# Rows of x turned on VectorE and carried through memory beside h, in two mixture-of-experts stages after chunked attention

## What is computed

```python
# N, D, E, F = 3072, 512, 8, 1024
top2 = argpartition(-noisy_logits, 2)[:, :2]          # first mixture
for e in range(E):
    for k in range(2):
        mask = top2[:, k] == e
        h = np.maximum(x[mask] @ w1[e], 0.0)
        out[mask] += top2_w[mask, k, None] * (h @ w2[e])
expert_idx = np.argmax(x @ w_gate, axis=1)            # second mixture, x = out of the first
for e in range(E):
    h = np.maximum(x[mask] @ w1[e], 0.0)
    out[mask] = gate_w[mask, None] * (h @ w2[e])
```

## Time and profile before

| | us |
|---|---|
| median of 3 runs | 1158.09 |
| lowest and highest run | 1156.57, 1162.1 |
| profiled execution, its own time | 1158.69 |
| its span in the trace | 1156.6 |

### The profile page before, as it was taken

The page is one execution under the profiler, slowest core; times in us unless marked ns, Lnnn a source line. Parts: engine busy times, 40 slices in busy tenths (PEclk is TensorE's granted clock), DMA queues, the critical chain, the costliest instruction groups (busy, mean ns, idle before and its releaser), DMA issues.

```text
span 1156.6 us, 29685 instructions
## 1 busy us (share of the span) xinstructions
PE 1085.6 (94%) x7939; PEld 879.6 (76%) x7940; DVE 643.4 (56%) x1360; ACT 280.0 (24%) x534; POOL 317.1 (27%) x473
## 2 busy tenths in 40 slices
PE   5989788999999999999999999989889999999995
PEld 4767566788888888888888888856668888878783
DVE  2767585655553552644635536317885246576861
ACT  3566321121212212121212122115211212121111
POOL 2004313332222232333322223220133223333321
PEclk9797889999999999999999999999999999999998
DMA  8998974877685774766867757559387447777952
GB/s 344 357 336 282 329 247 131 242 219 220 184 234 138 216 209 137 221 198 162 244 168 204 222 131 215 137 114 252 100 280 230 141 157 236 236 244 234 306 178 68
DMA packets 126990, 245.87 MB, mean 213 GB/s; under 512 B 17454, under 2 KB 70878, under 8 KB 126960
## 3 DMA queue, kind: packets, MB, share of 16 engines
q1 hardware_dynamic: 48608, 112.38, 28.9%
q10 hardware_dynamic: 61728, 90.25, 24.1%
q0 software_dynamic: 16624, 42.88, 16.7%
HBM read 169.51 MB, written 76.73 MB: 213 GB/s over the span
## 4 chain that ended last, share of the span: by engine, by line
PE 63%; DVE 7%; DMA 6%; issue 5%; DVEq 4%; ACT 1%; ACTq 1%; POOL 1%; POOLq 0%
PE moe_ps_y L1597 10%; PE moe_ps_y L1598 10%; PE moe_ps_y L1602 10%; PE moe_ps_h L1597 10%; PE moe_ps_h L1598 9%; PE moe_ps_h L1602 9%; DMA moe_h_moved<-h_d 3%; PE moe_ps_x L1590 3%; DVE weights L141 2%; DVEq L1478 2%; DMA moe_xg<-x_d,moe_from_row 2%; ACTq L1660 1%; DVE moe_h_lo L1710 1%; DVEq L141 1%; PE g_bank L343 1%
## 5 line engine op out<-in xcount | busy, mean ns | idle before, releaser
L1597 PE MATMUL moe_ps_h<-weights,moe_x_hi 128*128 (+1 forms) x640 | 253.1, 395 | 11.8 <-ACT moe_x_hi L1665 4.9
L1597 PE MATMUL moe_ps_y<-weights,moe_h_hi 128*128 (+1 forms) x624 | 251.5, 403 | 7.0 <-ACT moe_y L1685 3.4
L1598 PE MATMUL moe_ps_h<-weights,moe_x_hi 128*128 (+1 forms) x640 | 251.0, 392 | 0.0
L1598 PE MATMUL moe_ps_y<-weights,moe_h_hi 128*128 (+1 forms) x624 | 244.6, 392 | 0.0
L1710 DVE SCALAR_TENSOR_TENSOR moe_h_lo<-moe_h_moved,moe_h_hi 128x256 fp32r<-128x256 f32 x312 | 111.8, 422 | 231.2 <-ACT moe_h_hi L1674 231.2
L1674 ACT ACTIVATE moe_h_hi<-moe_h_moved 128x1024 fp32r<-128x1024 f32 x78 | 82.8, 1062 | 383.5 <-PE moe_ps_y L1602 313.9
L1602 PE MATMUL moe_ps_h<-weights,moe_x_lo 128*128 (+1 forms) x640 | 171.7, 390 | 0.0
L147 DVE TENSOR_TENSOR weights<-stage,weights (+1 forms) x128 | 156.8, 1225 | 19.7 <-DVE weights L141 19.2
L1602 PE MATMUL moe_ps_y<-weights,moe_h_lo 128*128 (+1 forms) x624 | 154.1, 389 | 0.0
L1597 PEld LDWEIGHTS moe_ps_h<-weights,moe_x_hi 128*128 128x128 f32 x640 | 121.2, 189 | 41.8 <-issue 15.3
L1597 PEld LDWEIGHTS moe_ps_y<-weights,moe_h_hi 128*128 128x128 f32 x624 | 117.8, 189 | 32.4 <-issue 7.1
(11 more groups left out here) (259 smaller groups left out, 861.8 us busy)
## 6 DMA issues: line engine op xcount, KB each, us to landing
stage<-in_w SPq DMA_DIRECT2D x128, 512.0 KB
h_d<-moe_h_turned ACTq DMA_DIRECT2D x80, 512.0 KB
moe_h_moved<-h_d ACTq DMA_DIRECT2D x320, 128.0 KB
v_sb<-in_v SPq DMA_DIRECT2D x24, 520.0 KB, 5.3
k_sb<-in_k SPq DMA_DIRECT2D x24, 512.0 KB, 6.3
x_d<-zero SPq DMA_DIRECT2D x27, 260.0 KB, 7.2
q_sb<-in_q SPq DMA_DIRECT2D x24, 256.0 KB, 4.5
x_d<-x_sb ACTq DMA_DIRECT2D x24, 256.0 KB, 6.0
```

The source lines that it names most:

```text
L1597: pe.matmul(out, a_hi, b_hi, start=(i == 0), stop=False)
L1598: pe.matmul(out, a_hi, b_lo, start=False, stop=False)
```

## The change

The transposes of x on TensorE are dropped from the loop. VectorE turns the rows of tile t+3 in 32x32 blocks from `xg` (`turn_x`) into the last four columns of a wider buffer `turned`, where the two turns of `h` of tile t+1 fill the first eight. The buffer in memory is laid out so that one DMA reads a whole tile back (`fetch`, 128 rows of 6 KB, before 4 x 128 pieces of 1 KB). It is written in four DMAs (`park`), two behind the first turn of h and two behind the second, each of 128 pieces of 1.5 KB. `high_x(t+2)` and `low_x(t+2)` read what `fetch(t)` brought, and `high_x` comes behind `park(t+1)` in ScalarE's order. The gathers run a tile or two further ahead. The first tiles of each mixture keep the transposes of before.

```diff
+TC = FC + DC
+LAG = 5
...
-        self.h_blocks = h_d.rearrange("(a p) (b r) -> b p a r", a=QB, b=QB)
+        self.parts = [h_d[b * QR:(b + 1) * QR, :].rearrange("p (a r) -> a p r", a=QB) for b in range(QB)]
...
-            self.h_turned = sb("h_turned", [P, QB, FC, QR])
-            self.h_moved = sb("h_moved", [P, QB, FC, QR])
+            self.turned = sb("turned", [P, QB, TC, QR])
+            self.moved = sb("moved", [P, QB, TC, QR])
...
-    def park(self, act, t):
+    def park(self, act, t, with_x=False):
...
-        act.wait_ge(s("turned"), t * 2 + 4)
         if not (isinstance(t, int) and t == 0):
-            act.wait_ge(s("moved"), t * (16 * QB))
-        act.dma_start(self.h_d, self.h_turned[:, :, :, :].rearrange("p b c q -> p (b c q)")).then_inc(s("parked"), 16)
...
+            act.wait_ge(s("moved"), t * 16)
+        if with_x:
+            act.wait_ge(s("xt_done"), t + 3)
+        n = TC if with_x else FC
+        for f in range(2):
+            act.wait_ge(s("turned"), t * 2 + (f + 3))
+            for b in (2 * f, 2 * f + 1):
+                act.dma_start(self.parts[b][:, :, 0:n * QR],
+                              self.turned[:, b, 0:n, :].rearrange("p c q -> p (c q)")).then_inc(s("parked"), 16)
...
-        act.wait_ge(s("parked"), t * 16 + 16)
+        act.wait_ge(s("parked"), t * (16 * QB) + 16 * QB)
         if not (isinstance(t, int) and t == 0):
             act.wait_ge(s("h_split"), t)
-        for b in range(QB):
-            act.dma_start(self.h_moved[b * QR:(b + 1) * QR, :, :, :].rearrange("p a c q -> p a (c q)"),
-                          self.h_blocks[b]).then_inc(s("moved"), 16)
...
+        if with_x:
+            act.wait_ge(s("x_split"), t + 2)
+        n = TC if with_x else FC
+        act.dma_start(self.moved[:, :, 0:n, :].rearrange("p a c q -> p a (c q)"),
+                      self.h_d.rearrange("p (a r) -> p a r", a=QB)[:, :, 0:n * QR]).then_inc(s("moved"), 16)
...
+        if moved:
+            act.wait_ge(s("moved"), t * 16 - 16)
+            act.wait_ge(s("l1_done"), t * 2)
+            act.nop(nofuse=True)
+            act.activation(self.x_hi[:, :, :].rearrange("p c (a q) -> p c a q", a=QB),
+                           self.moved[:, :, FC:TC, :].rearrange("p a c q -> p c a q"), ACT.Copy)\
+               .then_inc(s("x_high"), 1)
...
+    def turn_x(self, dve, t, second=False):
+
+        s, xg = self.s, self.xg_b if second else self.xg
+        if second:
+            dve.wait_ge(s("gathered_b"), 32)
+        else:
+            dve.wait_ge(s("gathered"), t * 16 - 16)
+        dve.wait_ge(s("parked"), t * (16 * QB) - 2 * 16 * QB)
+        dve.nop(nofuse=True)
+        dve.transpose(self.turned[:, :, FC:TC, :].rearrange("p b c q -> p c b q"),
+                      xg[:, 0:DM].rearrange("p (c b q) -> p c b q", c=DC, b=QB)).then_inc(s("xt_done"), 1)
...
             self.splits(dve, frm, mid)
+            if not first and not end:
+                self.turn_x(dve, t + 3)
             self.turn(dve, t + 1)
-            self.low_x(dve, t + 2)
+            if not end:
+                self.low_x(dve, t + 2, moved=not first)
+            if first:
+                self.turn_x(dve, t + 3, second=True)
             self.splits(dve, mid, to)
             self.low_h(dve, t, end)
...
-            self.high_x(act, t + 2)
-            self.park(act, t + 1)
+            if first:
+                self.high_x(act, t + 2)
+            self.park(act, t + 1, with_x=not end)
+            if not first and not end:
+                self.high_x(act, t + 2, moved=True)
             self.high_h(act, t, end=end)
             self.weigh(act, t - 1)
-            self.fetch(act, t + 1)
...
+            self.fetch(act, t + 1, with_x=not end)
...
             self.first_product(pe, t + 1)
-            self.x_transposes(pe, t + 2)
             self.second_product(pe, t - 1)
...
-    def pool_loop(self, pool, begin, m):
+    def pool_loop(self, pool, m):
...
+            self.scatter(pool, t)
+            pool.wait_ge(s("xt_done"), t + (LAG + 1))
             pool.nop(nofuse=True)
-            self.keep_gate(pool, t + 3)
-            self.gather(pool, t + 4)
-            self.scatter(pool, t)
...
+            self.keep_gate(pool, t + LAG)
+            self.gather(pool, t + (LAG + 1))
```

More of the change, by code:

```diff
@@ L611, in _ @@
             x.gather(pool, 0)
-            for t in range(1, EARLY):
-                pool.wait_ge(s("xt_done"), t)
-                x.keep_gate(pool, t - 1)
-                x.gather(pool, t)
+            x.gather(pool, 1, second=True)
+            pool.wait_ge(s("xt_done"), 1)
+            x.keep_gate(pool, 0)
+            x.gather(pool, 2)
+            pool.wait_ge(s("xt_done"), 2)
+            x.keep_gate(pool, 1, second=True)
             store_gates(2)
@@ L625, in _ @@
             x.scatter(pool, 0)
-            m = x.tiles(pool)
-            pool.wait_ge(s("xt_done"), EARLY + 1)
-            x.keep_gate(pool, EARLY)
-            x.gather(pool, EARLY + 1)
-            x.pool_loop(pool, 1, m)
+            m = x.gathered_ahead(pool)
+            pool.wait_ge(s("xt_done"), 4)
+            x.keep_gate(pool, 3)
+            x.gather(pool, 4)
+            x.gather(pool, 5, second=True)
+            pool.wait_ge(s("xt_done"), 5)
+            x.keep_gate(pool, 4)
+            x.gather(pool, 6)
+            pool.wait_ge(s("gathered_b"), 32)
+            x.keep_gate(pool, 5, second=True)
+            x.pool_loop(pool, m)
             pool.sem_inc(sem("x2_whole"), 1)
@@ L805, in _ @@
             ranks(2, NT)
-            x.x_transposes(pe, 1)
+            x.x_transposes(pe, 1, second=True)
             x.first_product(pe, 1)
@@ L1587, in x_transposes @@
         else:
-            pe.wait_ge(self.s("gathered"), t * 16 + (16 if isinstance(t, int) and t == 0 else self.gathers))
+            pe.wait_ge(self.s("gathered"), max(t, 1) * 16)
         for cc in range(DC):
@@ new lines, in high_x @@
+    def high_x(self, act, t, moved=False):
+        s = self.s
+        if moved:
[6 more added lines that the diff above has]
+        else:
+            act.wait_ge(s("xt_done"), t + 1)
+            act.activation(self.x_hi[:, :, :], self.ps_x[:, :, :], ACT.Copy).then_inc(s("x_high"), 1)
@@ L1686, in weigh, with low_x @@
            .then_inc(s("y_ready"), 1)
-    def low_x(self, dve, t):
+    def low_x(self, dve, t, moved=False):
         dve.wait_ge(self.s("x_high"), t + 1)
-        dve.tensor_tensor(self.x_lo[:, :, :], self.ps_x[:, :, :], self.x_hi[:, :, :].bitcast(F32), ALU.subtract)\
-           .then_inc(self.s("x_split"), 1)
+        if moved:
+            last = dve.tensor_tensor(self.x_lo[:, :, :].rearrange("p c (a q) -> p c a q", a=QB),
+                                     self.moved[:, :, FC:TC, :].rearrange("p a c q -> p c a q"),
+                                     self.x_hi[:, :, :].bitcast(F32).rearrange("p c (a q) -> p c a q", a=QB),
+                                     ALU.subtract)
+        else:
+            last = dve.tensor_tensor(self.x_lo[:, :, :], self.ps_x[:, :, :], self.x_hi[:, :, :].bitcast(F32),
+                                     ALU.subtract)
+        last.then_inc(self.s("x_split"), 1)
     def turn(self, dve, t):
@@ L1709, in low_h @@
             cols = slice(a * QR, (a + 1) * QR)
-            last = dve.scalar_tensor_tensor(out=h_lo[:, :, cols], in0=self.h_moved[:, a, :, :], scalar=0.0,
+            last = dve.scalar_tensor_tensor(out=h_lo[:, :, cols], in0=self.moved[:, a, 0:FC, :], scalar=0.0,
                                             in1=h_hi[:, :, cols].bitcast(F32), op0=ALU.max, op1=ALU.subtract)
@@ L1728, in vector_loop, with tile @@
         s, before, middle = self.s, self.routes.before, self.routes.middle
-        def tile(t, end=False):
+        def tile(t, first=False, end=False):
             frm, mid, to = self.counts(dve, t, (before, t), (middle, t), (before, t + 1))
@@ L1756, in scalar_loop, with tile @@
     def scalar_loop(self, act, begin, m):
-        def tile(t, end=False):
-            self.high_x(act, t + 2)
-            self.park(act, t + 1)
+        def tile(t, first=False, end=False):
+            if first:
[3 more added lines that the diff above has]
+                self.high_x(act, t + 2, moved=True)
             self.high_h(act, t, end=end)
             self.weigh(act, t - 1)
-            self.fetch(act, t + 1)
-        with act.Fori(begin, m) as t:
+            self.fetch(act, t + 1, with_x=not end)
+        tile(begin, first=True)
+        with act.Fori(begin + 1, m) as t:
             tile(t)
```

56 lines of the change are left out of this document (31 added, 25 removed).

## The result

The changed kernel takes 1650.06 us, the median of 4 runs (1649.2 to 1652.64). The kernel before took 1157.33 us beside it (4 runs, 1155.15 to 1162.1). The ratio is 1.4253, 95% interval 1.4209 to 1.4298. The forecast was 1191 with a range of 1143 to 1227. The sign was right, and the time was 459 us above the forecast.

The account below looks back on a forecast made before the run. TensorE was taken as the bound, at 11.35 us a first-mixture tile. Lost transposes against late parks and `high_x` gave +3 us in the first mixture and +30 in the second, on 1158.69: 1191, range 1143 to 1227.

Parts of the forecast that it names:

- What bounds the kernel, and what is removed: TensorE bounds each first-mixture tile at 11.35 us; dropping four transposes (0.44 us) leaves 10.9, 31 us over 70 tiles.
- The turn of x, `high_x`: VectorE's added block transpose of x costs 0.7 us; ScalarE's `high_x` from SBUF 0.60, 0.7 with waits.
- gated by `low_h` (+2.96): On ScalarE the next fetch goes out once VectorE's `low_h` ends, 2.96 us after a tile's first product.
- The fetch, 4.0 us: On ScalarE's queue, one DMA reading a tile takes 4.0 us from issue until the park, bounds 3.4 and 5.8.
- Four park issues, 1.8 us: Issuing the four writes of a park on ScalarE takes 1.8 us, bounds 1.4 and 1.8.
- A pair, 10.9 + 12.6: First-mixture tile with 1+2 weight pieces, then one with 1+0: 23.5 us together, before 22.7.
- The wider buffer: Half as many bytes again in both transfers: counted in the range, not in the sum.
- The tiles outside the two stretches, counted at nothing: Tiles outside the two mixture stretches are few and mostly keep their transposes, so they add nothing.
- forecast +3 and +30: Expected growth of the first and second mixture's stretches in us, from tiles with weight pieces against tiles without.
- The way through memory becomes the bound of every tile: Rival, chance 0.09: a fetch over 5.4 us bounds all tiles; at 5.8, +80 us, 1238.
- The last of the signs: If tiles without weight pieces take over 11.3 us, the fetch costs more than forecast.

Follow-up runs that it names:

- e6: The changed kernel with old-style transfers, x in its own buffer and transfers, `high_x` first on ScalarE, reads of x ahead of `weigh`: 1191.7 us.
- e1: The changed kernel with its four park writes cut by source rows (outermost count 32), all behind the second turn of h: 1347.21 us.
- e5: e2 with the park cut by block into four writes of outermost count 128, two behind each turn of h: 1399.16 us.
- e2: The changed kernel, x still carried, with the transfers of the kernel before: one write of 128 rows and four reads: 1297.06 us.
- e4: The kernel before, x turned on TensorE, with h alone written in four DMAs by source rows (outermost count 32) and read in one: 1161.28 us.
- e7: The kernel before with its write and four reads widened as if they carried x, the added columns unread zeros: 1190.87 us.
- e10: e12 in the first mixture, the kernel before in the second: 1326.44 us.
- e12: e13 with the turn of x also moved behind `low_x` and the write of x behind the write of h: 1389.27 us.
- e13: e6 with h written as 128 rows of 4 KB and the reads of x moved behind `weigh` and the reads of h: 1291.57 us.
- e14: e13 in the first mixture, the kernel before in the second: 1257.18 us.

## Why the prediction was wrong

**What bounds the kernel, and what is removed.** Right. Without the transposes TensorE needs 10.88 us a tile (e6, 10 tiles), forecast 10.9.

**The turn of x, `high_x`.** Right: 0.71 us for 0.7, and 0.63 for 0.6 to 0.7.

**The step that failed: a park's landing had no term.** The working took the next fetch as gated by `low_h` (+2.96), as in the earlier trace rows, and counted of the parks only their issues (1.8 us). In the kernel before the landing of one write is hidden there. In the change it takes 11.7 us from the first issue and is the longest part of the round. e1 puts it at 303 us of the 493, and e5, with its slower fetch, at 251. The shape was in the diff (`"p (a r) -> a p r", a=QB`), and I read it as "the pieces of the reads" when the reads have the outermost count 32.

**The fetch, 4.0 us.** In free tiles it measured 4.5 in the change, 5.1 in e1 and 7.0 in e2. In the second tiles of pairs it was 5.15, 6.4 and 8.55 (medians, from issue to the parks). My reason for 4.0 was that one DMA saves the 1.3 us of later issues. One DMA is faster than e2's four, but not by enough to reach 4.0. Its low bound of 3.4 comes to 3.5 from its own rows. The estimate of 3.8 us from the Trainium skill, "DMA: Bandwidth & Descriptors", section "Anatomy of one DMA", lies further off: the median landing in the changed kernel is 4.4. The Trainium skill fits that formula to DMAs that GpSimd issues, and the fetch is on ScalarE's queue.

**Four park issues, 1.8 us.** Measured 2.98 and 2.59 in the change, 2.64 in e1, 2.15 and 1.90 in e4's rows. The bound from four reads was too low.

**A pair, 10.9 + 12.6.** e1 has 12.9 + 15.8. In its first tile all four parks wait for the second turn and end at +11.4 in the median, forecast +9.95. In the second the mechanism was right: `high_x` is late, behind the late `low_h` and the parks. With e1's 6.4 for 4.0 and 2.25 for 1.8 the second tile comes to 12.6 + 2.4 + 0.45 = 15.45.

**The wider buffer.** It was in the range, at nothing in the sum. e7 measures 33 us, as much as my whole forecast of +33. That the forecast's size and this one agree is chance.

**The tiles outside the two stretches, counted at nothing.** The 47 whole tiles of the first stretch took 533.4 us before and 823.5 in the change, the 22 of the second 255.3 and 394.5. That is +290 and +139, forecast +3 and +30. The remaining 62 us lie outside, and so do some 13 us of e1's loss and of e7's.

**Rivals.** "The way through memory becomes the bound of every tile", with 0.09, is what happened, but not by the condition it was given. It wanted a fetch of over 5.4 us. The change's fetch took 4.5 in free tiles, and the landing of the parks did the rest. Its free tile of 11.3 us looks like e1's 11.4, which is luck in part: e1 has 5.1 for the fetch and 2.2 for the issues, the rival 5.8 and 1.8. The last of the signs, that free tiles above 11.3 us mean a dearer fetch, would have named the wrong transfer. Its 1238 is 109 us short of e1 and 412 short of the change. The ranges were bounds on single terms, and none covered a term that wasn't there.

**TensorE's busy time.** No step had a term for it. It grew by 97.2 us through the clock, below. In the tile above this didn't lengthen the round: although the matmuls were slow, h was turned by 607.54, and the parks could go only at 610.11. How much of the 97.2 us counts in other tiles wasn't measured.

## What to carry to other kernels

When a diff reshapes a DMA, read the outermost count of both sides before anything else, since four writes whose outermost count is 4 used a quarter of the engines and cost 251 to 303 us here (e5, e1). When an operand is put on a transfer that was hidden, follow the chain from that operand back to itself, over as many tiles as it takes, and sum landings as well as issues. The same sum should be made for each reordering: e10, e12, e13 and e14 each closed such a chain and lost 95 to 229 us against the kernel before, where a gain was expected.
